# Attention visits of a fused attention and MLP kernel moved to other slots of a chunk

## The reference, cut to what matters

```python
# attention, 4 batches, 8 heads, 576 positions, head size 64
scores = scale * q @ k.T                       # banded: window 32, plain for heads 0-3,
scores = where(mask, scores, -1e9)             # dilated by 4 for heads 4-7
x = (softmax(scores) @ v)                      # -> x: 4 x 576 x 512
# first MLP (token shift, squared relu, sigmoid gate)
xk = mu_k * x + (1 - mu_k) * x_prev
xr = mu_r * x + (1 - mu_r) * x_prev
x = sigmoid(xr @ w_r) * (relu(xk @ w_k) ** 2 @ w_v)
# second block: low-rank mix over tokens, then an MLP with 2048 hidden features
u = x + (U @ V over tokens)
out = u + relu(u @ w_ch1) @ w_ch2
```

## Time and profile before

| | |
|---|---|
| median of 3 runs | 767.17 us (765.24 to 768.49) |
| profiled execution | 767.08 us, its span 765.2 us |
| TensorE busy | 732.6 us (96%) |
| VectorE busy | 328.7 us (43%) |
| ScalarE busy | 299.2 us (39%) |
| GpSimd busy | 172.0 us (22%) |
| mean granted TensorE clock | 0.995 |

### The profile page before, as it was taken

The page is one execution under the profiler, slowest core; times in us unless marked ns, Lnnn a source line. Parts: engine busy times, 40 slices in busy tenths (PEclk is TensorE's granted clock), DMA queues, the critical chain, the costliest instruction groups (busy, mean ns, idle before and its releaser), DMA issues.

```text
span 765.2 us, 13125 instructions
## 1 busy us (share of the span) xinstructions
PE 732.6 (96%) x4860; PEld 640.9 (84%) x4860; DVE 328.7 (43%) x693; ACT 299.2 (39%) x803; POOL 172.0 (22%) x257
## 2 busy tenths in 40 slices
PE   4799989998999999999999999999999999999998
PEld 3678778887887787788899998999999899999997
DVE  6788676767676736634421312212131221213111
ACT  4786657676766566625441211111121111112110
POOL 6997120212121224214881000000000000000000
PEclk9999999999999999999999999999999999999999
DMA  7874545454454221001442102000110200011001
GB/s 142 198 183 88 108 107 117 86 108 106 103 102 104 69 66 56 1 29 56 138 143 37 42 1 42 19 23 10 31 41 0 41 23 18 10 31 42 0 1 42
DMA packets 165843, 49.00 MB, mean 64 GB/s; under 512 B 142880, under 2 KB 159776, under 8 KB 165792
## 3 DMA queue, kind: packets, MB, share of 16 engines
q1 hardware_dynamic: 129088, 43.99, 22.8%
q10 hardware_dynamic: 36704, 4.34, 3.7%
HBM read 34.98 MB, written 9.37 MB: 58 GB/s over the span
## 4 chain that ended last, share of the span: by engine, by line
PE 77%; ACT 9%; DVE 8%; issue 3%; ACTq 2%; DMA 1%; POOL 0%; DVEq 0%
PE bank L1361 24%; PE bank L1363 24%; PE bank L1362 24%; ACT probs L831 4%; ACTq L841 2%; PE bank L1419 2%; PE bank L1382 2%; DVE probs L1160 1%; DVE q_t L1098 1%; ACT L831 1%; ACT shifted L873 1%; DVE xf L1178 1%; PE bank L1510 1%; DVE neg_max L1132 1%; DVE probs L1122 1%
## 5 line engine op out<-in xcount | busy, mean ns | idle before, releaser
L1328 DVE SCALAR_TENSOR_TENSOR h_l<-bank,h_h 128x384 fp32r<-128x384 f32 x96 | 53.5, 557 | 289.9 <-ACT h_h L1059 289.8
L1059 ACT ACTIVATE h_h<-bank 128x384 fp32r<-128x384 f32 x96 | 47.2, 491 | 317.8 <-PE bank L1363 317.8
L1363 PE MATMUL bank<-ut_h,w_l 128*128 128x384 f32 x384 | 129.5, 337 | 0.0
L1361 PE MATMUL bank<-ut_h,w_h 128*128 128x384 f32 x384 | 129.3, 337 | 0.0
L1362 PE MATMUL bank<-ut_l,w_h 128*128 128x384 f32 x384 | 128.9, 336 | 0.0
L1363 PE MATMUL bank<-w_h,h_l 128*128 128x512 f32 x288 | 113.7, 395 | 0.0
L1362 PE MATMUL bank<-w_l,h_h 128*128 128x512 f32 x288 | 113.5, 394 | 0.0
L1361 PE MATMUL bank<-w_h,h_h 128*128 128x512 f32 x288 | 112.0, 389 | 0.0
L1361 PE MATMUL bank<-xs_h,wk_h 128*128 128x256 f32 x288 | 83.8, 291 | 0.2
L1362 PE MATMUL bank<-xs_l,wk_h 128*128 128x256 f32 x288 | 81.3, 282 | 0.0
L1363 PE MATMUL bank<-xs_h,wk_l 128*128 128x256 f32 x288 | 81.1, 282 | 0.0
(11 more groups left out here) (121 smaller groups left out, 1207.4 us busy)
## 6 DMA issues: line engine op xcount, KB each, us to landing
stage<-in_moe_w_ch_dram SPq DMA_DIRECT2D x16, 512.0 KB, 3.3
out_dram<-result SPq DMA_DIRECT2D x18, 256.0 KB, 2.0
u_tile<-result SPq DMA_DIRECT2D x80, 48.0 KB, 2.0
probs_dram<-probs_blocks SPq DMA_DIRECT2D x12, 240.0 KB, 2.0
probs_t<-probs_dram SPq DMA_DIRECT2D x36, 80.0 KB, 2.2
k_raw<-in_k_dram ACTq DMA_DIRECT2D x64, 40.0 KB, 2.3
q_raw<-in_q_dram SPq DMA_DIRECT2D x64, 40.0 KB, 2.1
q_raw<-in_q_dram SPq DMA_DIRECT2D x64, 32.0 KB, 2.1
```

The costliest lines, as they stand in the source:

```text
L1059: act.activation(h_h[:, m % KRING, :], h_bank[m % 2][:, 0:C2], ACT.Relu).then_inc(hh_done, 1)
L1328: dve.scalar_tensor_tensor(h_l[:, m % KRING, :], h_bank[m % 2][:, 0:C2], 0.0, h_h[:, m % KRING, :].bitcast(F32), op0=ALU.max, op1=ALU.subt ...
L1361: pe.matmul(dst, lhs[0], rhs[0], start=start, stop=False)
L1363: return pe.matmul(dst, lhs[1], rhs[0], start=False, stop=stop)
```

## The change

The tables give steps other slots. In `LATER` the visit of slot 4 goes to slot 3 (B of pair 0, D of pair 2), the other visits stay at 1, 6 and 9. A goes from slots 3, 5, 8, 0 to 2, 4, 7, 9, so that it is in a slot of its own or, for pair 3, ahead of the masks of slot 9. T of pair 0 goes from slot 6 to 5, the others stay. Parts 1 and 2 are written out in the same form. ScalarE runs its attention steps of slots 4 and 5 ahead of the sigmoids, in chunks 1 to 6; in slot 4 that is now the exponentials of pair 0. The shift of the third feature tile goes from slot 5 to slot 4.

```diff
-LATER = {"A": [-7, -5, -2, 0], "B": [-6, -4, -1, 1], "C": [-2, 0, 3, 5], "D": [-1, 1, 4, 6]}
+LATER = {"A": [-8, -6, -3, -1], "B": [-7, -4, -1, 1], "T": [-5, -2, 1, 3], "D": [-1, 1, 3, 6]}
 FIRST_ONE = {"A": [None, None, None, None], "B": [None, None, None, 4], "C": [None, 4, 5, 7], "D": [None, 5, 6, 8]}
-SECOND_ONE = {"A": [-5, -4, -2, 0], "B": [-4, -3, -1, 1], "C": [-2, 0, 3, 5], "D": [-1, 1, 4, 6]}
+SECOND_ONE = {"A": [-5, -4, -3, -1], "B": [-4, -3, -1, 1], "C": [-2, 0, None, None], "T": [None, None, 1, 3], "D": [-1, 1, 3, 6]}
 ...
-        for st in "ABCD":
-            n = (FIRST_ONE if k == 1 else SECOND_ONE if k == 2 else LATER)[st][p]
-            if n is not None:
-                SLOT_OF[st, k, p] = NUNIT * (k - 1) + n
-        if nth(k, p) >= MOVED_FROM:
-            del SLOT_OF["C", k, p]
-            SLOT_OF["T", k, p] = SLOT_OF["B", k, p] + 2
+        for st, slots in (FIRST_ONE if k == 1 else SECOND_ONE if k == 2 else LATER).items():
+            if slots[p] is not None:
+                SLOT_OF[st, k, p] = NUNIT * (k - 1) + slots[p]
 ...
-SHIFT_SLOT = [[4, 6, 7, 8]] + [[1, 2, 5, 7]] * (NC1 - 2)
+SHIFT_SLOT = [[4, 6, 7, 8]] + [[1, 2, 4, 7]] * (NC1 - 2)
 ...
                     else:
+                        if 0 < c < MIX_CHUNK:
+                            attention_slot(c * NUNIT + n)
                         wait(act, unit_mm, c * NUNIT + n + 1)
                         wait(act, x2_done, (c - 1) * T1 + m + 1)
                         act.activation(sig[:, m, :], unit_bank[n % 2][:, :], ACT.Sigmoid).then_inc(unit_out, 1)
 ...
                     if c < MIX_CHUNK:
-                        attention_slot(c * NUNIT + n)
+                        if c == 0 or kind == "k":
+                            attention_slot(c * NUNIT + n)
```

## The result

The changed kernel takes 778.55 us (median of 5 runs, 777.09 to 780.88) against 766.34 us (5 runs, 765.24 to 768.49) for the kernel before on the same chip: a ratio of 1.0159, interval 1.0132 to 1.0185. It is slower by 12.2 us. The prediction said 770.5, with 763.0 to 775.0 as its range. So the time lies outside the range, 3.6 us above its upper end.

What follows compares the result with a forecast made beforehand. TensorE was taken to set the time, with holes only in chunks carrying scores. Chunk 1 -1.2, chunks 3 and 5 -0.3 each, 2 and 4 +1.4 each, 6 +2.4: +3.4 on the 767.17 median, 770.5 us; range 763.0 to 775.0.

Steps and rivals of the forecast that it cites:

- The moved visit, probabilities: Step D of pair 2, slot 3: waits for probabilities through DRAM; net loss 1.0 us in long chunks, 1.5 in short.
- The moved visit, keys: Pair 0's scores, slot 3: wait 1.3 to 1.4 us for turned keys, inside D's wait; lower bound 0.9 net.
- Exponentials ahead of both sigmoids: ScalarE, slot 4: hidden with 3 us to spare; table load moves before pair 1's exponentials, priced at 1.28 us.
- rival 5: ScalarE's table switch before pair 1's exponentials costs 2.66 us; 777.5 us in all; chance 0.03.
- The end of a chunk: Visit of slot 6 to next k0: VectorE takes over; gain 1.3 us in long chunks, 0.15 in short ones.
- Chunk 6: No scores there; step D can start at 11.15 us, wanted at 8.75: 2.4 lost on a TensorE without holes.
- Chunk 1: Its wait of 1.14 us becomes about 1.25, net 0.1; its end gains 1.3: -1.2 in all.
- The clock: TensorE's granted clock: entered as unchanged in the sum, with changes to it left to other cases.
- rival 3: TensorE's two clock falls, 1.5 us each, go with the waits of slot 9: 767.5 us, no change; chance 0.15.
- rival 4: New clock falls on TensorE in chunks 6, 2 and 4: slower still, 772.5 to 775 us; chance 0.12.
- Rival 2: Chunk ends: TensorE's waits vanish whole because VectorE does not set the end; faster, 764.4 us; chance 0.17.

Runs made afterwards that it cites:

- the repeat: The changed kernel run again, unaltered, on the chip of the other follow-up kernels: 776.81 us, ratio 1.0173 to the kernel before.
- the second experiment: Changed kernel with step D of pair 2 and its shift put back from slot 3 to slot 4: 768.62 us, ratio 1.0026 to the kernel before.
- the fourth experiment: Changed kernel with step D of pair 2 back in slot 4 in chunk 6 alone: 775.38 us, ratio 1.0112 to the kernel before.

## Why the prediction was wrong, step by step

The direction of the sum (a small loss) came out, and so did the waits that it named. The time came out 8 us above it for two reasons: most terms of the sum were too small, and the clock was entered as unchanged. Taking out of each chunk's change what the lower clock cost (one less the granted clock, microsecond by microsecond, in both kernels), the orders differ by -0.3, +2.8, +0.5, +2.5, +0.2 and +2.6 us in chunks 1 to 6: +8.3 where the sum said +3.4. In chunks 2 to 5 the moved visits came out 1.8 above the forecast and the ends of the chunks 2.1, by the two parts of a chunk used above. The rest of the 11.7 us, 3.4, is clock, and in this execution all of it is the fall in chunk 0, as those of the other chunks cancel against the two of the kernel before. The lengths that were named beforehand came out as 37.84 for chunk 3 (forecast 37.1), 37.46 for chunk 4 (36.4) and 34.12 for chunk 6 (near 34).

**The moved visit, probabilities: right, too small.** The scores stood where forecast (10.15 after the chunk's start in chunk 4, forecast 10.0). The product started at 11.52 instead of 11.15: the last of the three reads landed 2.48 after it went out, where I took 2.2 from the earlier trace rows, the median of all such reads, and the product started 0.14 after the landing, which I had not counted. In the six moved visits the last read took 2.31 to 2.66. The two waits together, with the restart of the pipeline after each, were 1.76, 2.36 and 1.69 in chunks 3, 4 and 5 (forecast 1.5, 2.0, 1.5), and 2.75 in chunk 2, which I had priced like chunk 4. There the reads go out 0.19 later behind the write and the last takes 0.18 longer, while the transfers of V are under way; that these are the reason is not tested. I had asked what follows the write in SyncE's queue and not what stands ahead of it, and I had not looked at chunk 2 by itself. In the profiled execution the loads of V were issued just in time; in the repeat and in the second experiment they held the write 0.2 and 0.8 after the end of T.

**The moved visit, keys: right.** Waits of 1.05 to 1.33, forecast 1.3 to 1.4, and the larger part of the two in all chunks but 2. The second experiment shows that they are a cost of their own: without the DMA's wait this visit still loses.

**Exponentials ahead of both sigmoids: right at nothing.** The order put back left chunk 4 at 37.44. The table costs what the earlier trace rows show, 1.28 and not 2.66: ScalarE after, at pair 1's exponentials,

```profile
218.63 1.28 ACT L827 ACT_TABLE_LOAD   x1
219.93 0.35 ACT L827 ACTIVATE probs<-probs,neg_max 128x64 f32<-128x64 f32 x1
```

so rival 5 is out. But the load is no longer hidden. Before, it stood between the sigmoids and pair 0's exponentials, ahead of the visit of slot 6; now it stands behind that visit, on the way to the mix. In chunk 4 the mix of the last tile starts 7.47 after the visit, with early turns alone 6.86 and before 6.89. The prediction had this as a term (7.35), and no run takes the load away alone.

**The end of a chunk: right in kind, mis-sized most.** I gave it a gain of 1.3 in long chunks and 0.15 in short ones. Measured from the visit of slot 6 to k0: 16.32 in chunk 3 (forecast 15.9, before 17.22), a gain of 0.9; 15.21 in chunk 4 (forecast 14.5, before 14.67), a loss of 0.5; 14.90 in chunk 2 (before 14.45), again a loss of 0.5. The wait moved where I said, from the keys to the square's low part, and was 0.78 in chunk 2 and 1.37 to 2.05 in the others, where I said about 1. The row of VectorE work from the mix to the low part of xk took 6.62 in chunk 3 and 6.11 in chunk 4, forecast 6.29 and 5.55. In chunk 4 it is as long as before (6.12), though its hole of 0.57 is gone; with the mix 0.6 later, that makes the loss. Part of the row is the pair of squares, 1.76 against the 1.4 that I had read. In chunk 2 the row took 5.54, as forecast, but the low part of xk then took 1.75 instead of 1.21. The turn of pair 3, which I had taken at the price of the turn that it replaces, gave 0.43 and 0.42 back when it was moved behind the edge. GpSimd's part in it is read from rows and not tested: 0.97 for the square beside GpSimd, 0.42 for one in slot 3. The Trainium skill, "SBUF — State Buffer", section "SBUF: two separate sides", says that a VectorE instruction with two SBUF inputs and a GpSimd one that reads SBUF lock each other out for a whole instruction; the rows agree in direction.

**Chunk 6: right.** 2.6 (forecast 2.4), and the fourth experiment takes all of it away.

**Chunk 1: wrong.** Forecast -1.2, measured -0.3 without the clock and +1.1 with it. The miss is its end, which waits 2.05: without the clock it gained about 0.5 where I said 1.3. Its moved visit waits 1.12 for keys and, which I had left out, 0.56 more for the DMA.

**The clock: the step that failed beside the sizes.** The prediction held it where it was, and split the other cases over rival 3 (the falls go with the waits of slot 9, 767.5) and rival 4 (new falls, 772.5 to 775). The waits of slot 9 did go, and the falls behind them in chunks 1 and 5 went with them, but falls behind the new waits came: the mean clock over nine runs was 0.991, where the kernel before had 0.995. Of 777 us, 0.004 is 3.1 us, and filling the waits gave 2.1 to 3.9 back. Rival 4 is the one that came true. It had a chance of 0.12 and looked for the falls in chunks 2, 4 and 6, while the profiled execution has them in chunks 0 and 1 and the repeat in 1 and 6; and its price stood on top of a sum that was itself 5 too low; the two together are why the range did not reach. Rival 2 is out for the changed kernel: VectorE's row, which starts when ScalarE's shift is there, does set the end.

The Trainium skill, "TensorE: Matmul & The Clock Gate", section "A second HAM failure mode: psum-queue depth-cycling", tells of a kernel in which short and frequent idle times between groups of matmuls brought the clock down and up. The runs agree as far as they go: waits of 1 to 2 us, several in a chunk, with a mean clock that came back when they were filled. Why a fall follows one such wait and not the next stays open. Waits of 1.33 and 0.91 in chunk 4 had none, 1.12 and 0.56 in chunk 1 had one. Which chunks get them differs between executions of one kernel.

What else is open: the share of the VectorE row's 0.5 us that is GpSimd's, what the table load behind the visit of slot 6 costs by itself, and whether the changed order of visits would pay with keys turned still earlier. That was not tried.

## What to carry to other kernels

Move the turn, not its user: preparing data one slot ahead of a waiting consumer won 7.9 us (some 5 of it waits, the rest clock), while pulling the consumer ahead as well shortened the time that a 5.4 us round trip through DRAM had, and made 19.6 us of waits out of 12.0. When a step is moved on an in-order queue, look for each chunk by itself at what stands ahead of its transfers, and never move it in a chunk that has no hole to fill (2.6 us here for nothing). On TensorE count the waits that a change makes, not only their lengths: one of 1 to 2 us can bring a stretch at half the clock besides, which here was about a quarter of the loss.

## What the runs showed of the hardware

- A stretch of three to four microseconds at the lower clock costs 1.5 to 1.8 us: chunk 1 of the kernel before was 40.35 with one and 38.55 without, and its chunk 5 was 1.49 longer than chunk 3 with the same work. Over the executions of one kernel the span follows the mean granted clock by 0.9 us for 0.001.
- Idle matmuls in the waits bring the mean clock from 0.991 to 0.998 and from 0.995 to 0.999. They did not make the kernel before slower, with more work to do; that they made it faster (2.2 us at the median, ratio 0.9957 to 1.0001) is not clear of noise.
- The same waits can bring a fall in one execution and none in the next. In chunk 0, just ahead of 40 us, TensorE waits 0.6 and 1.0 in the changed kernel, 0.5 and 1.0 in its repeat, and 0.4 and 1.0 in the kernel before; only the first of the three shows a fall there (0.50 from 40 to 46 us, about 3 us lost).
- Three reads behind a write that are wanted at once took 3.44 us from the first one's issue to the product in chunk 4, 0.4 more than issue gap and median landing of such reads give (0.84 + 2.2): the last one took 2.48 to land, and the product started 0.14 after that.
- A load of the exponential table took 1.28 us in every trace, and the next activation, where its input was there, began 0.01 to 0.02 after its end (218.63 + 1.28, exponentials at 219.93).
